# Attention and two MoE blocks on one core: how the row reciprocals reach the output, and how the batches are looped

## The reference, cut to what matters

```python
B, H, S, D = 4, 8, 576, 64
scores = q @ k.T / sqrt(D) + min(-(cum_i - cum_j), 0)      # cum: running sum of max(s, 0)
scores = where(causal, -1e9, scores)
scores = scores - max(scores, axis=-1)
attn = exp(scores); attn = attn / (sum(attn, axis=-1) + 1e-9)
x = (attn @ v)  -> (B * S, H * D)                          # 2304 tokens, 512 wide
xn = x / sqrt(mean(x * x) + 1e-6) * rms_g
x = (silu(xn @ w_gate) * (xn @ w_val)) @ w_out             # 512 -> 1536 -> 512
h = x @ w_in; out = (h - tanh(h)) @ w_out2                 # 512 -> 2048 -> 512
```

## Time and profile before

| | |
|---|---|
| median of 3 runs | 1107.44 us (1105.72 to 1108.49) |
| profiled execution | 1111.58 us |
| its span, first to last instruction | 1109.8 us |
| PE matmul busy | 1080.0 us, 97% |
| DVE busy | 444.0 us, 40% |
| ACT busy | 418.7 us, 38% |
| POOL busy | 168.4 us, 15% |
| mean granted TensorE clock | 0.99 |

### The profile page before, as it was taken

One profiled execution on the slowest core, in us unless ns is written; L12 is line 12 of the kernel. 1 busy time (PEld: TensorE's weight loads), 2 busy tenths in 40 slices (PEclk: granted clock), 3 DMA queues, 4 the chain that ended last, 5 costly groups with the idle time before them and its releaser, 6 DMA issues.

```text
span 1109.8 us, 19419 instructions
## 1 busy us (share of the span) xinstructions
PE 1080.0 (97%) x6836; PEld 998.6 (90%) x6836; DVE 444.0 (40%) x1214; ACT 418.7 (38%) x1030; POOL 168.4 (15%) x178
## 2 busy tenths in 40 slices
PE   4999999899999999999999999999999999999998
PEld 3888787789999999999999999999999999899997
DVE  6677677554432321321322333433223232332322
ACT  4676667664422232222222233433223232332322
POOL 4777777730000000000000000000000000000000
PEclk9999999899999999999999999999999999999999
DMA  5444455213200000000000122310000000000000
GB/s 187 150 150 150 154 157 152 85 32 96 67 1 1 1 0 0 0 0 0 0 0 0 29 76 77 95 29 29 1 1 29 0 28 0 0 28 0 28 0 28
DMA packets 48452, 51.66 MB, mean 47 GB/s; under 512 B 2990, under 2 KB 38830, under 8 KB 48394
## 3 DMA queue, kind: packets, MB, share of 16 engines
q1 hardware_dynamic: 48394, 50.94, 14.8%
HBM read 41.63 MB, written 4.87 MB: 42 GB/s over the span
## 4 chain that ended last, share of the span: by engine, by line
PE 95%; issue 1%; DVE 1%; DMA 1%; POOL 1%; ACT 1%; SPq 0%; ACTq 0%; DVEq 0%; POOLq 0%
PE HP L954 15%; PE HP L956 15%; PE HP L955 15%; PE YP L955 11%; PE YP L956 11%; PE YP L954 11%; PE TP L892 5%; PE OP L908 5%; PE SC L879 4%; PE OP L920 2%; PE SC L880 2%; DMA Qraw<-in_qT 0%; ACT PT L451 0%; DMA QO<-QA 0%; PE MP L927 0%
## 5 line engine op out<-in xcount | busy, mean ns | idle before, releaser
L954 PE MATMUL HP<-XS,WA 128*128 128x384 f32 x576 | 194.6, 338 | 0.3 <-ACT AC L518 0.3
L956 PE MATMUL HP<-XS,WA 128*128 128x384 f32 x576 | 193.0, 335 | 0.0
L955 PE MATMUL HP<-XS,WA 128*128 128x384 f32 x576 | 192.7, 335 | 0.0
L760 DVE TENSOR_TENSOR AC<-AC,HP 128x384 f32<-128x384 f32 (+2 forms) x78 | 40.3, 523 | 294.1 <-PE HP L956 294.1
L811 DVE TENSOR_TENSOR AC<-HP,AC 128x384 f32<-128x384 f32 (+1 forms) x108 | 54.3, 512 | 216.3 <-ACT AC L580 216.3
L580 ACT ACTIVATE AC<-HP 128x384 f32<-128x384 f32 x96 | 47.2, 492 | 215.7 <-PE HP L956 215.2
L954 PEld LDWEIGHTS HP<-XS,WA 128*128 128x128 f32 x576 | 108.2, 188 | 3.0 <-issue 0.5
L955 PEld LDWEIGHTS HP<-XS,WA 128*128 128x128 f32 x576 | 108.2, 188 | 2.4
L956 PEld LDWEIGHTS HP<-XS,WA 128*128 128x128 f32 x576 | 108.1, 188 | 0.0
L518 ACT ACTIVATE AC<-HP 128x384 f32<-128x384 f32 x72 | 35.4, 492 | 178.3 <-PE HP L956 178.3
L954 PE MATMUL YP<-HS,WX 128*128 128x384 f32 (+2 forms) x312 | 102.1, 327 | 0.5 <-DVE HS L766 0.5
(11 more groups left out here) (109 smaller groups left out, 2029.3 us busy)
## 6 DMA issues: line engine op xcount, KB each, us to landing
X<-in_w SPq DMA_DIRECT2D x52, 256.0 KB, 3.3
Kraw<-in_kT SPq DMA_DIRECT2D x16, 576.0 KB, 4.8
Qraw<-in_qT SPq DMA_DIRECT2D x16, 576.0 KB, 5.6
out_rows<-OS SPq DMA_DIRECT2D x18, 256.0 KB, 2.2
QO<-QA SPq DMA_DIRECT2D x15, 288.0 KB, 3.3
Vt<-in_v SPq DMA_DIRECT2D x16, 256.0 KB, 3.1
WRAW<-in_w SPq DMA_DIRECT2D x16, 256.0 KB, 2.8
Vt<-in_v SPq DMA_DIRECT2D x16, 32.0 KB, 2.1
```

Of the source, the lines that this page charges most:

```text
L760: dve.tensor_tensor(AC[:, m % 2, cols], AC[:, m % 2, cols], HP[:, 1, cols], ALU.mult).then_inc(prod_done if part is None else prod_part, 1)
L954: pe.matmul(dst, w(0), x(0), start=start, stop=False)
L955: pe.matmul(dst, w(0), x(1), start=False, stop=False)
L956: return pe.matmul(dst, w(1), x(0), start=False, stop=stop)
```

## The change

The padding columns of PR no longer hold zeros: a new ACT instruction, `pad`, fills them with the row's reciprocal. The transpose of the first key block then carries them into rows 0 to 63 of PT, where they meet V's zero rows and add nothing. A DMA per half (`load_rb`) copies those 64 rows from PT to RB, which gets three buffers. The spread matmuls and the copy from PSUM go. The transposes now wait for pad, PT's first copy of a step waits for the RB transfers of two steps before, and `output` waits for RB's transfer and moves behind `recip` in DVE's order. All batches are written out. In the prologue, K and Q of pair 1 are loaded ahead of the decay rows, memsets move from DVE to POOL, and the zeroing of PR and the filling of RR go. SP's per-pair loads are placed at fixed steps of the pair. POOL's wait on the QO copy goes.

```diff
-T_LAG, V_LAG = 2, 3
-R_LAG = 2
+T_LAG, V_LAG, O_LAG = 2, 3, 4
+RBS = 3
+ALL = B * STEPS
...
+def evacuated(n, hh):
+
+    g = groups_of(n, hh)[0][0]
+    return g % 2, g // 2 + 1
...
-        RB = sb("RB", [P, 2, P], F32)
+        RB = sb("RB", [P, RBS, P], F32)
...
+            def load_rb(n):
+
+                z = q_block(n % QB)[1]
+                wait(sp, o_evac, n - RBS + 1)
+                for hh in range(2):
+                    engine, count = evacuated(n, hh)
+                    sp.wait_ge((evac_act, evac_dve)[engine], count)
+                    sp.dma_start(RB[hh * D:(hh + 1) * D, n % RBS, 0:z], PT[0:D, n % 2, hh, 0:z]
+                                 ).then_inc(rb_in[n % RBS], 16)
+
             load_qk(0, 0, 0)
+            load_qk(0, 1, 1)
...
-            load_qk(0, 1, 1)
...
-            def load_ahead(b, p, last=False):
-
-                at, after = (b + (p + 1) // PAIRS, (p + 1) % PAIRS), (b + (p + 2) // PAIRS, (p + 2) % PAIRS)
-                if not last or p + 1 < PAIRS:
-                    wait(sp, scores_done, 2 * (b * STEPS + QB * p))
+            for n in range(ALL):
+                k, u = n // QB, n % QB
+                at, after = divmod(k + 1, PAIRS), divmod(k + 2, PAIRS)
+                if u == 0 and k + 1 < B * PAIRS:
+                    wait(sp, scores_done, 2 * QB * k)
                     load_decay(*at)
-                    sp.wait_ge(q_hi, 2 * (b * PAIRS + p + 2))
+                if n >= T_LAG:
+                    load_rb(n - T_LAG)
+                if u == 1 and k + 1 < B * PAIRS:
+                    sp.wait_ge(q_hi, 2 * (k + 2))
                     load_qo(*at)
-                if not last or p + 2 < PAIRS:
-                    if isinstance(b, int) and b * PAIRS + p == 0:
-                        sp.wait_ge(qo_first, 2)
-                        sp.wait_ge(klo_first, 2)
-                        sp.wait_ge(qlo_first, 2)
-                    else:
-                        sp.wait_ge(k_lo, 2 * (b * PAIRS + p))
-                        sp.wait_ge(q_lo, 2 * (b * PAIRS + p))
-                    load_qk(*after, p % 2)
-                if not last or p + 1 < PAIRS:
-                    wait(sp, pv_done, b * STEPS + QB * p)
-                    load_v(*at, at[1] % 2)
-                if not last or p + 2 < PAIRS:
-                    sp.wait_ge(w_lo, b * PAIRS + p + 1)
-                    load_weights(*after)
-
-            for p in range(PAIRS):
-                load_ahead(0, p)
-            with sp.Fori(1, B - 1) as b:
-                for p in range(PAIRS):
-                    load_ahead(b, p)
-            for p in range(PAIRS):
-                load_ahead(B - 1, p, last=True)
+                    if k + 2 < B * PAIRS:
+                        if k == 0:
+                            sp.wait_ge(qo_first, 2)
+                            sp.wait_ge(klo_first, 2)
+                            sp.wait_ge(qlo_first, 2)
+                        else:
+                            sp.wait_ge(k_lo, 2 * k)
+                            sp.wait_ge(q_lo, 2 * k)
+                        load_qk(*after, k % 2)
+                if u == 3 and k + 1 < B * PAIRS:
+                    wait(sp, pv_done, QB * k)
+                    load_v(*at, (k + 1) % 2)
+                if u == 2 and 0 < k < B * PAIRS - 1:
+                    sp.wait_ge(w_lo, k)
+                    load_weights(*at)
+            for n in range(ALL - T_LAG, ALL):
+                load_rb(n)
...
+            pool.wait_ge(consts, 2)
+            for j in range(2):
+                pool.memset(QO[D:D + 2, j].bitcast(F32), 1.0).then_inc(padded, 1)
+            for j in range(2):
+                pool.wait_ge(padded, j + 2)
+                pool.memset(Vt[0:P - PAD, j, 0, :], 0.0).then_inc(padded, 1)
+            pool.wait_ge(padded, 4)
...
-                pool.wait_ge(qo_in[j], 16 * (2 * b + p // 2 + j))
...
+            pool.memset(onesm[:], 1.0 / DM).then_inc(onesm_set, 1)
+            pool.memset(eps[:], RMS_EPS).then_inc(onesm_set, 1)
+            for b in range(B):
+                batch(b, last=(b == B - 1))
...
+                        if ks[0] == 0 and b * STEPS + n >= 2:
+                            before = b * STEPS + n - 2
+                            act.wait_ge(rb_in[before % RBS], 2 * 16 * (before // RBS + 1))
...
-            def spread_out(b, n):
+            def pad(b, n):
+
                 z = q_block(n % QB)[1]
-                act.wait_ge(spread_mm, b * STEPS + n + 1)
-                act.activation(RB[:, n % 2, 0:z], OP[:, n % 2, 0:z], ACT.Copy).then_inc(spread_done, 1)
+                act.wait_ge(recip_done, b * STEPS + n + 1)
+                act.activation(PR[0:z, n % 4, :, 0:PAD], RR[0:z, n % 4].rearrange("p (h o) -> p h o", o=1).broadcast_to([z, 2, PAD]), ACT.Copy
+                               ).then_inc(pad_done, 1)
...
-                    if n > R_LAG or not first:
-                        spread_out(b, n - R_LAG - 1)
                     if last and n == ROOT_STEP:
                         root(0)
                     for hh in range(2):
                         if n >= T_LAG or not first:
                             evacuate(b, n - T_LAG, hh)
                         exponential(b, n, hh)
+                        if hh == 0 and (n >= 1 or not first):
+                            pad(b, n - 1)
...
-            for j in range(4):
-                dve.memset(PR[:, j, :, 0:PAD], 0.0).then_inc(padded, 1)
-            dve.memset(RR[:], 1.0).then_inc(padded, 1)
             dve.memset(RS[:, :, :, 1:2], SUM_EPS).then_inc(eps_set, 1)
-            for j in range(2):
-                dve.memset(QO[D:D + 2, j].bitcast(F32), 1.0).then_inc(padded, 1)
-            for j in range(2):
-                dve.memset(Vt[0:P - PAD, j, 0, :], 0.0).then_inc(padded, 1)
...
-                dve.wait_ge(pv_done, b * STEPS + n + 1)
-                dve.wait_ge(spread_done, b * STEPS + n + 1)
+                step = b * STEPS + n
+                dve.wait_ge(pv_done, step + 1)
+                dve.wait_ge(rb_in[step % RBS], 2 * 16 * (step // RBS + 1))
                 dve.tensor_tensor(X[:, p, bass.ds((b + turn) * S + q0, z)], OP[:, n % 2, 0:z],
-                                  RB[:, n % 2, 0:z], ALU.mult).then_inc(o_evac, 1)
+                                  RB[:, step % RBS, 0:z], ALU.mult).then_inc(o_evac, 1)
...
-                    if n > V_LAG or not first:
-                        output(b, n - V_LAG - 1)
                     for hh in range(2):
                         minima(b, n, hh)
-                        if hh == 0 and (n >= 1 or not first):
-                            recip(b, n - 1)
+                        if hh == 0:
+                            if n >= 1 or not first:
+                                recip(b, n - 1)
+                            if n >= O_LAG or not first:
+                                output(b, n - O_LAG)
...
-                pe.wait_ge(exp_done, b * 2 * STEPS + 2 * n + hh + 1)
+                pe.wait_ge(pad_done, b * STEPS + n + 1)
...
-                pe.wait_ge(spread_done, b * STEPS + n + 1)
+                wait(pe, o_evac, b * STEPS + n - 1)
...
-            def spread(b, n):
-
-                z = q_block(n % QB)[1]
-                pe.wait_ge(recip_done, b * STEPS + n + 1)
-                wait(pe, o_evac, b * STEPS + n - 1)
-                pe.nop(nofuse=True)
-                for hh in range(2):
-                    last = pe.matmul(OP[hh * D:(hh + 1) * D, n % 2, 0:z],
-                                     RR[:, n % 4, hh:hh + 1].broadcast_to([P, D]), ident[:, 0:z],
-                                     start=True, stop=True)
-                last.then_inc(spread_mm, 1)
...
-                    if n >= R_LAG or not first:
-                        spread(b, n - R_LAG)
```

More of the change, by code:

```diff
@@ L212, in build @@
         eps_done = sem("eps_done"); recip_done = sem("recip_done")
-        spread_mm = sem("spread_mm"); spread_done = sem("spread_done")
+        pad_done = sem("pad_done"); rb_in = [sem(f"rb_in{i}") for i in range(RBS)]
         t_done = sem("t_done"); evac_act = sem("evac_act"); evac_dve = sem("evac_dve")
@@ L502, in _ @@
                 act.activation(QO[0:D, 0, hh], Qraw[0:D, 0, hh], ACT.Copy).then_inc(qo_first, 1)
[L503 to L509, removed]
-                    for hh in range(2):
-                        evacuate(B, n - T_LAG, hh)
+            for b in range(B):
+                batch(b, first=(b == 0), last=(b == B - 1))
+            pad(B, -1)
+            for n in range(T_LAG):
+                for hh in range(2):
+                    evacuate(B, n - T_LAG, hh)
             def silu(c, m):
@@ L642, in _ @@
                                      ).then_inc(cum_step, 1)
-            dve.memset(onesm[:], 1.0 / DM).then_inc(onesm_set, 1)
-            dve.memset(eps[:], RMS_EPS).then_inc(onesm_set, 1)
             def minima(b, n, hh):
@@ L680, in evacuate @@
                         wait(dve, pv_done, b * STEPS + n - 1)
```

(27 more changed lines are left out.)

## The result

The changed kernel takes **1120.08 us** (median of 4 runs, 1114.19 to 1123.64), the kernel before, beside it, 1106.95 (4 runs, 1105.72 to 1108.49). The ratio is 1.011, with a 95% interval of 1.0084 to 1.0137: it is slower by about 13 us, where 15 us less were predicted. The profiled execution took 1114.19 us (span 1112.4), at the low end of its runs.

A forecast was written before the change was run, and what follows sets the result against it. PE was taken as the main bound, with DVE as full in blocks 3, 4 and 0. Savings of 4.2 + 3.1 + 6.6 + 0.5 + 0.8 = 15.2 us, transfers costing 0, gave a median of 1092; forecast 1086 to 1097, range 1078 to 1104.

The forecast's parts named there:

- Transfers: New DMAs from PT to RB on SP's queue: land in 2.1 us, cost 0, range up to 1 us per pair.
- evac(2,0): Copy to PT of query block 2, half 0: needs block 0's transfer, forecast with about 1 us to spare.
- Rival B: RB transfers wait behind big loads in SP's queue: about 0.7 us more per pair, 1102 us; chance 0.20.
- Rival C: Block 2's transfer lands late, holding a later PT copy: each us over 2.3 costs one per pair, 1117; chance 0.08.
- The steady part: Pairs outside prologue and tail: removing spread matmuls saves 0.3 us per pair, 4.2 us over 14 pairs.
- T(3,1): Transposes of query block 3, half 1: forecast 5.60 us after block 3's scores, not 5.40, held by DVE's list.
- evac(2,1): DVE's copy to PT of query block 2, half 1: empties the PSUM half T(3,1) needs, which starts 0.15 us later.
- Rival A: PE is the only bound: the spreads' 19 us come in full, 1077 us; chance 0.12.
- The pad: ACT instruction replacing the RB copy, in ACT's queue before the transposes: taken as 0.33 us, no more counted.
- The prologue: Kernel start: earlier K and Q of pair 1 save 6.6 us, first scores 0.5 us earlier.
- Rival D: Kernel start: prologue does not gain, POOL's first split of pair 1 behind 14 us; 1099 us, chance 0.12.
- The loop edge: Batch loop's one jump back: writing batches out saves 2.1 + 1.0 = 3.1 us.

The follow-up runs named there:

- e1: Changed kernel without the transfers into RB and the waits for them, RB filled with ones, so no division by the row sum: 1093.83 us, ratio 0.987.
- e3: Changed kernel with later pairs' K and Q loads issued by ACT on its own queue, at the start of block 1's step: 1108.05 us, ratio 0.9999.
- e8: Changed kernel without K and Q loads from pair 2 on (old K and Q reused), all RB transfers kept: 1098.21 us, ratio 0.991.
- e4: Kernel before with batches written out and the new prologue; spread matmuls stay, no pad or RB transfers: 1098.24 us, ratio 0.9915.
- e7: e1 with the output moved back to the start of DVE's step: 1089.1 us, ratio 0.9844.
- e6: Kernel before with the new prologue alone, batch loop kept: 1100.7 us, ratio 0.9952.
- e5: Kernel before with the batches written out and nothing else: 1104.47 us, ratio 0.999.
- e9: Changed kernel with each pair's K and Q loads cut into four pieces of 288 KB, in the steps of blocks 1 to 4: 1109.6 us, ratio 1.0028.

## Why the prediction was wrong
**The step that failed** is *Transfers*: "I take 2.1, nearest in size, so it just fits; cost 0, range up to 1 us per pair", and with it "about 1 us to spare" for block 0. It is a mis-sized term, and large enough to turn the sign: 26 us (e1), about 1.8 per pair. Two numbers in it were wrong.
- *The landing time.* The 2.1 us came from a 32 KB load whose median holds no big load beside it. Where nothing is beside them, the transfers do land in 1.7 to 1.9 us. Block 0's stand beside 1.15 MB and take 4.5 us in the median, 5.03 in the chain.
- *The end of K and Q.* "So they end near 91.7" was 89.0 plus a shift of 2.7. The shift was about right. K's issue in the kernel before, and in the changed one with the scores of block 1 ahead of it:
```profile
84.21 0.35 SPq L255 DMA_DIRECT2D Kraw<-in_kT  x1
...
101.22 0.35 PE L896 MATMUL SC<-KA,QA 128*128 128x192 f32 x1
...
104.92 0.53 SPq L262 DMA_DIRECT2D Kraw<-in_kT  x1
```
From the scores of block 1 it was 84.21 - 83.36 = 0.85 us and is 104.92 - 101.22 = 3.70, 2.9 later, and 3.70 or 3.71 in nine pairs of the trace. (In the pair of the chain above it is 90.52 - 85.36 = 5.16: PE ran at the lower clock there while SP waited for block 4's copies.) The end was not right: at 89.0 the mean share of the DMA engines fell, but Q, issued at 84.68, has a median landing of 5.6 us in the kernel before too, which makes 90.3, and with the shift 93.2. That leaves nothing before "shortly before 93.42", instead of about 1 us to spare.

In the pair of the chain block 0's transfer, needed at 97.70 - 2.54 = 95.2, lands at 97.6, and that is the worst; the other waits before evac(2,0) are 0.4 to 2.4 us. A late transfer also pushes back what follows: from the scores of block 0 to those of block 1 are 85.36 - 81.07 = 4.29 us there, 2.32 before. What the forecast had no term for is the clock: behind two of PE's stands it fell to the lower level, which makes some 3.5 of the 20 us between pairs 2 and 13.

**Rival B** had the place right (block 0's transfer, ACT before a PSUM copy, seen as an ACT wait that ends with a DMA into RB) and the price wrong: 0.7 per pair, where 1.8 were measured. Its range ended at 1104, 16 us short. The rule that its sentence rests on, from the Trainium skill (DMA: Bandwidth & Descriptors, Queues, rings and completion order), that one issuing queue's descriptors are taken in ring order, agrees with the changed kernel's chain, where the small transfer lands some 0.9 us after the estimated end of the big ones. e3 shows that it isn't the whole: behind no big load in its own queue, a transfer still took 6.7 us. The same page (Rules for kernel authors) says that spreading DMAs over issuing engines gives no bandwidth, since all of them run on the same 16 DMA engines; e3's 409 GB/s at a share of 1.08 agrees, beside 401 in the changed kernel (94 to 95 us, share 1.01).

**Rival C**, slower through block 2's transfer, had the right side, and its 1117 us come near the measured time by luck: in the changed kernel no wait is in its place. With the K and Q loads gone its wait does appear, six times, for at most 4.4 us (e8).

**What held.**
- The steady part in its sum, not in its steps. A pair takes 13.11 us in e4 (34.74 to 178.92 for 11 pairs) and 12.64 in e1: spreads and pad bring 0.47 per pair, where 0.3 was taken. The scores of block 3 to T(3,1) are 5.32 us, where 5.60 was predicted and 5.40 stood before: the output in its new place costs nothing there (e7). T(3,1) starts 0.23 us behind evac(2,1) in both e1 and e7, which agrees with DVE's list as the bound of blocks 3 and 4, but no run shortened that list before it. Rival A (PE is the only bound, 1077) falls: even without transfers the time is 1093.8. Spreads, pad and the copy off ACT are worth 4.4 us together with the tail (e1 less e4), not 19.
- The pad: 0.29 to 0.30 us in the timeline, 0.33 taken.
- The prologue: pair 1 starts at 22.87 with no PE gap before it, POOL's first split of pair 1 begins at 9.65 and the first scores at 10.41 (10.9 predicted). Rival D falls: its sign was a split behind 14 us. The size was 5.2 us (e6), not 7.1. The 6.6 was read from the profiled execution, which at 1111.58 us was slower than every timed run beside it, and whose clock was 0.50 for 6 us there; e5, with the same old prologue, had 0.60 and then 0.83 in 26 to 32 us. A term for low clock that is read from one slow execution can be too large; how much of the 1.9 us this explains is not shown.
- The loop edge: the gap near 120 us is gone, as said, but e5 measures about 1 us for it where 3.1 were counted, while the traces have 3 us or more at that pair. This stays open.

Without the transfers' term the forecast of 1092 stands 1.7 us from e1's 1093.83. Part of that is luck: the steady part gave more than counted, prologue and loop edge measured alone gave less, and e1 lost 2.3 us to a lower clock near 200 us that neither e4 nor e7 shows to that extent.

## What to carry to other kernels
A small transfer on which the engines wait is priced by what else the DMA engines have in hand when it is issued, not by its size or its median landing; look at the DMA share of that stretch, and recount when the big loads are issued once the small ones stand ahead of them in the queue. If a burst can't be avoided, moving it only chooses which small transfer is late: give the small ones a buffer and a step of slack instead, until the worst landing fits. Count the clock as well: where TensorE stands for the late transfer, it may run at its lower level afterwards. And put an in-order engine's deferrable work into the gap in which it waits anyway; one output in the wrong place was worth 0.15 us per pair here.

## What the hardware showed that was not expected
- A queue of its own doesn't protect a small transfer: with K and Q on ACT's queue the largest landing on SP's was 6.7 us, against 6.0 with all on one queue. The Trainium skill (DMA: Bandwidth & Descriptors, Queues, rings and completion order) says that a DMA engine takes turns between queues packet by packet, and also that a DMA's semaphore increment lands only after all earlier writes of that engine, from every queue. By the first, a transfer on its own queue should pass most of the load; by the second, it wouldn't. e3 shows the lateness, and no run here tells which of the two made it.
- SP needs 0.46 us or more to issue one RB transfer (two in a row took 1.11 us at 106.45 in the changed kernel), more than the 0.3 taken in the prediction.
- Much of the spread between runs of one kernel goes with TensorE's granted clock. The changed kernel's four runs are 1114.19 us at a mean clock of 0.995, 1118.82 at 0.993, and 1121.34 and 1123.64 at 0.989; e9's fastest and slowest are 1105.49 at 0.998 and 1126.55 at 0.982. A clock of 0.016 less over 1100 us is about 18 us of full-speed work (an estimate), of 21 between those two. Four runs of e7 at 0.998 lie within 0.9 us.
